# A gated linear attention and two channel mixers: first loads in another order, more identity products at the start

## The reference

```python
for t in range(S):                      # per batch and head, state is D x D
    state = alpha[:, :, t, :, None] * state + einsum('bhd,bhe->bhde', k[:, :, t], v[:, :, t])
    y[:, :, t] = einsum('bhd,bhde->bhe', q[:, :, t], state)
x = y.transpose(0, 2, 1, 3).reshape(B, S, 384)
h = relu(x^T @ w_tok1) @ w_tok2         # 768 -> 256 -> 768, over steps
u = x + h^T
x2 = u + relu(u @ w_ch1) @ w_ch2        # 384 -> 1536 -> 384
xk, xr = mixes of x2 with x2 one step earlier (mu_k, mu_r)
out = sigmoid(xr @ w_r) * (relu(xk @ w_k)**2 @ w_v)
```

## Time and profile before

| | |
|---|---|
| median of 3 runs | 744.44 us (744.19 to 745.77) |
| the profiled execution | 746.56 us, of which the span from first to last instruction is 744.8 us |
| TensorE busy in the span | 735.3 us |
| VectorE, ScalarE, GpSimd busy | 462.3, 333.1, 189.3 us |
| mean granted TensorE clock | 0.998 |

### The profile page before, as it was taken

One profiled execution on the slowest core, in us unless ns is written; L12 is line 12 of the kernel. 1 busy time (PEld: TensorE's weight loads), 2 busy tenths in 40 slices (PEclk: granted clock), 3 DMA queues, 4 the chain that ended last, 5 costly groups with the idle time before them and its releaser, 6 DMA issues.

```text
span 744.8 us, 13733 instructions
## 1 busy us (share of the span) xinstructions
PE 735.3 (99%) x4598; PEld 725.2 (97%) x4598; DVE 462.3 (62%) x1283; ACT 333.1 (45%) x942; POOL 189.3 (25%) x339
## 2 busy tenths in 40 slices
PE   8999999999999999999999999998999999999998
PEld 7899999999999999999999999998999999999998
DVE  6988878764977873887874312337365374473661
ACT  4865544432444442544443231336364373463551
POOL 2874545341224433223434340010000000000000
PEclk9999999999999999999999999999999999999999
DMA  9874433421424331242430033010011110110000
GB/s 203 199 141 98 89 49 69 58 38 40 56 37 58 69 52 27 55 57 39 83 66 1 32 100 124 33 33 33 32 43 42 43 33 32 53 42 32 11 21 32
DMA packets 174026, 43.81 MB, mean 59 GB/s; under 512 B 161297, under 2 KB 171153, under 8 KB 173969
## 3 DMA queue, kind: packets, MB, share of 16 engines
q1 hardware_dynamic: 170720, 37.98, 25.7%
q0 software_dynamic: 1152, 4.72, 1.7%
q10 hardware_dynamic: 2096, 0.39, 0.3%
HBM read 33.63 MB, written 9.44 MB: 58 GB/s over the span
## 4 chain that ended last, share of the span: by engine, by line
PE 92%; DVE 3%; ACT 3%; issue 1%; DMA 1%; SPq 0%; DVEq 0%; ACTq 0%
PE bank L719 20%; PE bank L735 20%; PE bank L812 14%; PE bank L790 12%; PE bank L799 4%; PE bank L636 4%; PE bank L613 4%; PE bank L707 3%; PE bank L675 3%; PE bank L640 2%; PE bank L643 2%; PE bank L698 1%; PE bank L608 1%; PE bank L604 1%; PE bank L585 1%; PE bank L687 1%
## 5 line engine op out<-in xcount | busy, mean ns | idle before, releaser
L897 ACT ACTIVATE hid_hi<-bank 128x384 fp32r<-128x384 f32 x96 | 47.2, 492 | 117.5 <-PE bank L719 117.5
L1151 DVE SCALAR_TENSOR_TENSOR hid_lo<-bank,hid_hi 128x384 fp32r<-128x384 f32 x96 | 53.3, 555 | 68.3 <-ACT hid_hi L897 65.0
L994 ACT ACTIVATE relu_k<-bank 128x384 f32<-128x384 f32 x64 | 31.5, 491 | 102.8 <-PE bank L790 85.2
L719 PE MATMUL bank<-u_hi,wch_hi 128*128 128x384 f32 x288 | 71.7, 357 | 0.0
L719 PE MATMUL bank<-u_lo,wch_hi 128*128 128x384 f32 x288 | 65.9, 336 | 0.0
L735 PE MATMUL bank<-hid_lo,wch_hi 128*128 128x384 f32 x288 | 65.6, 335 | 0.0
L719 PE MATMUL bank<-u_hi,wch_lo 128*128 128x384 f32 x288 | 65.4, 334 | 0.0
L735 PE MATMUL bank<-hid_hi,wch_hi 128*128 128x384 f32 x288 | 65.4, 334 | 0.0
L735 PE MATMUL bank<-hid_hi,wch_lo 128*128 128x384 f32 x288 | 65.3, 334 | 0.0
L500 POOL TENSOR_SCALAR_AFFINE_SELECT relu_k<-relu_k 128x256 f32<-128x256 f32 x72 | 29.3, 407 | 127.1 <-ACT relu_k L879 127.1
L1271 DVE TENSOR_TENSOR x_half<-bank,x_half 128x384 f32<-128x384 f32 x24 | 13.4, 557 | 77.6 <-PE bank L812 77.6
(11 more groups left out here) (124 smaller groups left out, 1814.3 us busy)
## 6 DMA issues: line engine op xcount, KB each, us to landing
w_raw<-in_moe_w_ch SPq DMA_DIRECT2D x12, 384.0 KB, 3.8
x_scratch<-x_half POOLq DMA_DIRECT2D x8, 576.0 KB, 3.5
out<-x_half SPq DMA_DIRECT2D x24, 192.0 KB, 1.9
vt<-in_v SPq DMA_DIRECT2D x48, 72.0 KB, 2.2
qka<-in_q SPq DMA_DIRECT2D x49, 48.0 KB, 2.2
qka<-in_alpha SPq DMA_DIRECT2D x49, 48.0 KB, 2.2
qka<-x_scratch SPq DMA_DIRECT2D x4, 577.5 KB, 3.7
qka<-in_k SPq DMA_DIRECT2D x48, 48.0 KB, 2.2
```

Source lines behind the costliest of these rows:

```text
L719: mm = nc.tensor.matmul(dst, ch1_w(a, n % KC, jj), u[c][:, n % KC, half * HT:(half + 1) * HT], start=(n == 0), stop=(n == 3 * KC - 1))
L897: nc.scalar.activation(dst, b_ring[t % 2][:, 0:HT], func).then_inc(tile_hi, 1)
L994: nc.scalar.activation(relu_k[:, j % 2, :], b_ring[j % 2][:, 0:HT], ACT.Relu)\
L1151: ins = nc.vector.scalar_tensor_tensor(dst, src, 0.0, hi, ALU.max, ALU.subtract)
```

## The change

Three edits. The load of alpha for the last three pairs of chunk 0 moves from SP's queue to ACT's, where v of chunk 0 stood, and v of chunk 0 moves to SP's queue behind q. The first weight piece is issued behind q, k and alpha of chunk 1, the second behind those of chunk 2, and the third behind v of chunk 2; before, the first two stood ahead of chunk 1 and the third ahead of chunk 2. And the identity products go from 4, 2, 1, 1, 1, 1, 1 to 10, 7, 2, 3, 3, 3, 2, that is from 11 to 30.

```diff
@@ SP
-            for n, t in ((0, q), (2, alpha)):
-                sp.dma_start(qka3[0][n][:, 2:H, 0:D], t[0, 2:H, 0:P, :].rearrange("h p d -> p h d"))\
-                  .then_inc(qka_loaded[0], 16)
-            for c in range(3):
-                if c > 0:
-                    load_qka(c)
-                    load_v(c)
-                for n in range(2 * c, min(2 * c + 2, NRAW)):
-                    load_piece(n)
+            sp.dma_start(qka3[0][0][:, 2:H, 0:D], q[0, 2:H, 0:P, :].rearrange("h p d -> p h d"))\
+              .then_inc(qka_loaded[0], 16)
+            load_v(0)
+            for c in range(1, 3):
+                load_qka(c)
+                load_piece(c - 1)
+                load_v(c)
+            load_piece(2)
@@ TensorE
-            WARM = (4, 2, 1, 1, 1, 1, 1)
+            WARM = (10, 7, 2, 3, 3, 3, 2)
@@ ACT
-            act.dma_start(qka3[0][1][:, 2:H, 0:D], k[0, 2:H, 0:P, :].rearrange("h p d -> p h d"))\
-               .then_inc(qka_loaded[0], 16)
-            act.dma_start(vt3[0].rearrange("p (h d) -> p h d", h=H),
-                          v[0, :, 0:P, :].rearrange("h p d -> p h d")).then_inc(v_loaded[0], 16)
+            for n, t in ((1, k), (2, alpha)):
+                act.dma_start(qka3[0][n][:, 2:H, 0:D], t[0, 2:H, 0:P, :].rearrange("h p d -> p h d"))\
+                   .then_inc(qka_loaded[0], 16)
```

## The result

The changed kernel takes 747.35 us at the median of 7 runs (746.84 to 747.99), the kernel before 744.94 at the median of 7 (744.19 to 746.46): a ratio of 1.0028 with a 95% interval of 1.0017 to 1.0040. That is 2.4 us slower, on the slow side of the 0.2% bound, and above the range of 743.4 to 746.8. Its profiled execution took 747.14 us, with a span of 745.4. Two executions in the sets further down, 756.83 us of the kernel before and 764.25 us of a variant, had a lower mean granted clock (0.98 and 0.971) and stand in no median or comparison here.

What follows compares the result with a forecast made beforehand. TensorE was taken as the bound, 92% of the chain; loads 0 and products +0.5 us gave 747.1 against the profiled 746.56, or 744.9 us on the median 744.44. Range 743.4 to 746.8.

Steps and rivals of the forecast that it cites:

- the rule (R + 10.31) / 2: End of step 1's transposes if TensorE's clock rises at R; with R taken as 6.8 it gave 8.56.
- Slots of three products: TensorE's slots 4 and 5, three products where one stood: 2.15 us each against 1.71.
- the loads were put at 0: Start of the kernel: alpha's earlier load gains 0, covered by 17 products; the other moved loads cost 0.
- the spread of q: Slot 3: step 1's scores need q spread, taken as done 2.2 us after that step's transposes, before 2.36.
- The extra 0.45 to 1 us: Start of the kernel: alpha landing 0.45 to 1 us earlier, a gain only with the old products.
- The loss of 0.5: First scan of step 6 at 18.00 against 17.46, a loss of 0.54, rounded to +0.5 us and kept.
- Set on the median: 744.9: The +0.5 us put on the median of the kernel before, 744.44, giving 744.9 us.
- goes or comes: Rival near 520 us: the clock drop, worth 1.7 us, may vanish, giving 743.2; chance 0.10 beyond 0.2%.
- the late rise: Rival at step 1's transposes: clock rises as late as before, R about 10.2, +2.2 us, 746.6 us; chance 0.15.
- Theory A: Experiments' theory: the clock's rise at the start moves between executions, and the profiled one of before was late.
- C: Experiments' theory: the clock drop near 520 us comes in some executions of before, more of the changed kernel's.
- B: Experiments' theory: the difference of 2.4 us arises outside what the head's trace shows.

Runs made afterwards that it cites:

- spread splits: Three of four low w_v splits done earlier by VectorE, behind tiles 3, 5 and 7: 742.36 us on the kernel before, 743.44 on the changed kernel.
- the splits on GpSimd: Three of four low w_v splits moved from VectorE to GpSimd: 746.35 us on the kernel before, 746.75 on the changed kernel.

## Why the prediction was wrong

**Right: the mechanism of the head and its sizes.** With the rise at 5.7, the rule (R + 10.31) / 2 gives 8.01 for the end of step 1's transposes, 0.56 behind the old 7.45; the scans of step 1 measure the same shift at 0.58 (7.72 and 8.30). Both ends were read some 0.2 us too early: rows 2 give the old transposes 0.87 and not 0.64, until 7.68, and the new ones end at 8.27. Slots of three products were put at 2.15 us, measured 2.16; the loads were put at 0 under the new products, and with the old loads the time is the same (747.50 and 747.35). The scan of step 6 came at 17.86, forecast 18.00 for R = 6.8 and 17.45 for R = 5.7, so the sum was 0.4 too low there. 0.24 of it is the spread of q: from 8.01, the end by the prediction's own reckoning, to the scores of step 1 at 10.45 it is 2.44 us, near the old 2.36 and not the 2.2 taken. 0.15 is in these scores (0.70 in place of 0.55). That a shift of the scan is kept is shown by the table. The extra 0.45 to 1 us that the loads would bring if uncovered is 0.95 at the scan of step 6 in the profiles (16.51 and 17.46), 1.05 at the medians with spread splits, and 1.3 at the medians where the drop comes and goes. The weight pieces moved as well, so how much of it is the other queue and how much the pieces behind it, no run separates.

**Wrong, the first step: one execution stood for before.** The loss of 0.5 was counted from the profiled execution, whose rise came near 11.5 and whose handover stood at 17.46, and between the two profiled executions it was met: 747.1 forecast, 747.14 measured. The step that failed is the next one, "Set on the median: 744.9": it put the same +0.5 on the median of before, and nothing for the drop; the medians lie 2.4 apart. The four profiles of kernels with before's head hand over at 17.46, 17.47, 17.00 and 16.52, mean 17.1; the four with the changed head, old or new loads, at 17.86, 18.12, 17.88 and 18.79, mean 18.2. For executions without a profile the handover can be estimated from the table, as the span less 727.5 with a drop and less 725.9 without: 17.1 at the median of the 68 of before (16.4 to 18.7), 18.1 for the 7 of the changed kernel (17.6 to 18.8). With the late wait gone the medians say the same, 743.44 against 742.36; only with the splits on GpSimd is it 0.4 to 0.5. So the start costs some 1.0 us, not 0.5. By this estimate the profiled execution of before handed over 0.3 later than the median one, that of the changed kernel 0.3 earlier. Before's rise is often earlier than the one I had seen, and then, as I read it, the 10 and 7 products, which hold step 1 until 7.8 or later, buy nothing back.

**Wrong, the second step: the set on the median, and the drop as a rival of one sign.** I saw the drop near 520, called it one that "goes or comes", priced only its going, and set the sum on before's lower median as if nothing else changed. The runs show the drop in 27 of 68 executions of before (745.6 to 748.0, median 746.4; the other 41 at 744.2 to 745.3, median 744.65; by set 15 of 27, 8 of 26 and 4 of 15), in all 7 of the changed kernel and in all 10 of the one with only its products. The two kernels with all the new products never escaped it; with the eight late products taken away it came in 5 of 12. Its price of 1.6 us times the 0.6 more of the executions is 1.0 us. Start and drop together make 2.0 of the 2.4 us; the rest is within the interval of 0.9 us on either side. The seven executions of before in the result divide it in the same way: the changed kernel's 747.35 lies 1.15 above the middle one of the three with the drop (746.20), and the other 1.26 is that the median of before, 744.94, falls among the four without.

**Its place among the rivals.** The time fell beyond the case that I called the late rise (746.6), but the rise was not late: 5.7. The right sign on that side had the wrong mechanism. Theory A alone gives some 1.0 of the 2.4 us, C as much again; B is refused by the table, in which nothing but the wait and the drop changes the time behind the handover.

**What stays open.** Why the drop follows the wait in every execution of the changed kernel. TensorE stood still for 2.1 us each time, in kernels that dropped and in those that didn't, and the distance from the start of the kernel to the wait differs by 0.5 us only. With the late products taken away the drop became rarer (5 of 12), and shorter waits never brought it (0 of 36, and 0 of 27 with none), so it hangs on the wait and, as it seems, on the head; through what, no run here shows. It may also be that 17 of 17 overstates it, since the share in the kernel before itself went from 4 of 15 to 15 of 27 between sets. The share of the rises at each place isn't known either: only the profiled executions show theirs, and the handover doesn't tell of it alone (17.46 and 17.47 with rises more than 1 us apart).

## What to carry to other kernels

Profile the kernel before more than once where a change is worth less than 1%, and look at what differs between executions: here a clock drop of 1.6 us came and went behind one wait of 2.1 us, and a change at the other end of the kernel went with a drop in every execution. Work that only keeps an engine busy belongs where the engine would otherwise wait for data; the ten products held step 0 until 5.9, 2 us beyond its data, and the seven held step 1 until 7.8, again 2 us beyond, and the clock did not give that back. The better change lay elsewhere: spreading three splits into VectorE's slack takes out the wait and the drop, and with the new loads and the old products gives 741.3 us, 0.5% below before.

## What was not expected of the hardware

- VectorE's elementwise product of 128x384 float32 in SBUF takes 0.56 us alone and 1.81 to 1.83 beside a subtraction of 128x768 on GpSimd (1.83 to 1.87). It ends 0.41 us behind GpSimd's (514.88 + 1.83 = 516.71 and 514.43 + 1.87 = 516.30). The Trainium skill (GPSIMD Engine Reference, Specifications) says that GpSimd's SBUF interfaces are shared with VectorE, with contention for instructions of two SBUF inputs; the trace agrees.
- One standstill of TensorE of 2.1 us was enough for the granted clock to fall to 0.50 for 3.4 us, in some executions and not in others, with the same rows around it. Behind waits of 1.1 us it came in none of 36 executions.
- At the start of every profiled execution, the granted clock of the windows reads 1.00 while a product takes 0.43 us in place of 0.22: the column doesn't show the low clock there, only the durations do.
- The rise came near 5.7 (changed) to 7.5 (changed, spread splits) with the new products. With the old ones it came near 10 to 11.5 in five of seven profiles, and before the transposes of step 1 in two, before with spread splits (by 6.62) and the new loads with the splits on GpSimd (by 6.00). With products 6 and 3 on the new loads it came near 5.0 in both profiles.
